# Attention, dense layer and routed experts in one launch: filler matmuls around the routing, and a new order of transposes and low parts in the expert tiles

## The reference

```python
do_compute = (x @ w_skip) > 0            # the other rows pass through
e_idx = np.argmax(xc @ w_gate, axis=1)   # xc: the rows that compute
h = np.maximum(xc[mask] @ w1[e], 0.0)    # 512 -> 1024
y[mask] = gate_w[mask, None] * (h @ w2[e])   # 1024 -> 512
out[do_compute] = xc + y
```

## Time and profile before

| | |
|---|---|
| median of 3 runs | 961.71 us |
| profiled execution | 961.93 us |
| its span | 960.1 us, so 1.8 us lie around it |
| mean granted TensorE clock | 0.959 |
| busy: TensorE, VectorE, ScalarE, GpSimd | 92%, 89%, 69%, 72% |

### The profile page before, as it was taken

The page is one execution under the profiler, slowest core; times in us unless marked ns, Lnnn a source line. Parts: engine busy times, 40 slices in busy tenths (PEclk is TensorE's granted clock), DMA queues, the critical chain, the costliest instruction groups (busy, mean ns, idle before and its releaser), DMA issues.

```text
span 960.1 us, 19356 instructions
## 1 busy us (share of the span) xinstructions
PE 882.6 (92%) x6322; PEld 721.0 (75%) x6322; DVE 854.0 (89%) x1708; ACT 661.8 (69%) x1297; POOL 694.4 (72%) x891
## 2 busy tenths in 40 slices
PE   3566799999999999999999999999999994999996
PEld 1344577888888888888888888888878983777875
DVE  6999999999999998999999999999980237888888
ACT  3677677777787677676778677777764223877875
POOL 2899798877777776787778787778785544566664
PEclk9867699999999999999999999999999995999999
DMA  8964333464354657867436544353343935555970
GB/s 317 376 215 129 118 118 120 157 203 157 115 176 167 192 162 231 241 191 240 136 119 187 169 162 162 127 187 125 132 133 126 333 117 216 200 213 184 337 279 10
DMA packets 69083, 174.76 MB, mean 182 GB/s; under 512 B 20898, under 2 KB 26018, under 8 KB 64624
## 3 DMA queue, kind: packets, MB, share of 16 engines
q1 hardware_dynamic: 67136, 168.39, 52.2%
q0 software_dynamic: 1840, 5.06, 1.6%
HBM read 153.66 MB, written 20.75 MB: 182 GB/s over the span
## 4 chain that ended last, share of the span: by engine, by line
PE 80%; DVE 12%; POOL 2%; issue 2%; ACT 2%; ACTq 0%; DMA 0%; SPq 0%; DVEq 0%; POOLq 0%
PE psum L1188 7%; PE psum L1190 7%; PE psum L1189 7%; PE psum L1128 7%; PE psum L1148 7%; PE psum L1205 7%; PE psum L1206 7%; PE psum L1207 6%; PE psum L1167 6%; DVE top L925 5%; DVE left L931 5%; PE psum L1334 2%; PE psum L1309 2%; PE psum L1131 2%; PE psum L1315 2%
## 5 line engine op out<-in xcount | busy, mean ns | idle before, releaser
L925 DVE MAX8 top<-left 128x8 f32<-128x576 f32 x432 | 305.3, 750 | 0.0
L931 DVE MATCH_REPLACE8 left<-top,left 128x576 f32<-128x576 f32 x288 | 212.1, 745 | 0.0
L565 POOL TENSOR_TENSOR s_sb<-s_sb,below 128x576 f32<-128x576 f32 x144 | 203.3, 1430 | 2.3 <-ACT below L721 2.3
L1188 PE MATMUL psum<-x_high,w_in_high 128*128 128x256 f32 x576 | 169.4, 294 | 1.6 <-POOL x_low L571 1.1
L1190 PE MATMUL psum<-x_high,w_in_low 128*128 128x256 f32 x576 | 163.8, 284 | 0.0
L1189 PE MATMUL psum<-x_low,w_in_high 128*128 128x256 f32 x576 | 163.7, 284 | 0.0
L712 ACT ACTIVATE s_sb<-psum 128x576 f32<-128x576 f32 x144 | 93.5, 650 | 88.6 <-PE psum L1128 72.5
L580 POOL TENSOR_TENSOR square<-relu 128x256 f32<-128x256 f32 x144 | 88.5, 615 | 88.2 <-ACT relu L754 87.7
L1128 PE MATMUL psum<-k_sb,q_sb 64*128 64x288 f32 x512 | 107.2, 499 | 29.6 <-ACT s_sb L712 24.4
L585 POOL TENSOR_TENSOR g_low<-square,g_high 128x256 fp32r<-128x256 f32 x144 | 107.8, 749 | 35.2 <-POOL square L580 27.0
L721 ACT ACTIVATE below<-s_sb,steep_kth 128x576 f32<-128x576 f32 x144 | 110.8, 770 | 29.8 <-POOL neg_max L553 29.8
(11 more groups left out here) (174 smaller groups left out, 1795.3 us busy)
## 6 DMA issues: line engine op xcount, KB each, us to landing
w_ring<-w_split SPq DMA_DIRECT2D x144, 512.0 KB, 4.5
weights<-w SPq DMA_DIRECT2D x32, 1024.0 KB
v_sb<-v_main SPq DMA_DIRECT2D x48, 256.0 KB, 2.6
w_split<-w_ring SPq DMA_DIRECT2D x16, 512.0 KB, 3.8
k_sb<-kT SPq DMA_DIRECT2D x32, 144.0 KB, 4.7
k_sb<-kT SPq DMA_DIRECT2D x32, 128.0 KB, 4.5
q_sb<-qT SPq DMA_DIRECT2D x32, 128.0 KB, 4.3
weights<-w_out SPq DMA_DIRECT2D x1, 4096.0 KB, 13.2
```

The costliest lines, as they stand in the source:

```text
L565: nc.gpsimd.tensor_tensor(s_sb[:, s % SBUFS, n, 0:S], s_sb[:, s % SBUFS, n, 0:S], below[:, n, :], ALU.subtract).then_inc(masked, 1)
L925: v.max(top[:, par, n, r, :], src).then_inc(topk_step, 1)
L931: v.match_replace(left[:, n, :], top[:, par, n, r, :], src, LOWEST).then_inc(topk_step, 1)
L1188: t_.matmul(dst, wh, x_high[:, j % 2, k, :], start=k == 0, stop=False)
```

## The change

It has three parts. `keep_busy(n)` issues n products of 128x128 by 128x512 into PSUM bank 4, which nothing reads; it is called at six places around the routing with 3, 2, 6, 16, 12 and 10. In an expert tile, TensorE transposes hidden half 0 first, then the next tile's rows, then hidden half 1; VectorE makes the low part of w2 piece 2 between the low parts of hidden half 0 and half 1. Before tile 0, VectorE makes the rows' low part ahead of w1 piece 2.

```diff
             def routed_tile(s):            # VectorE
-                for ff in range(3):
-                    split_w2_low(s, at, ff)
+                split_w2_low(s, at, 0)
+                split_w2_low(s, at, 1)
                 place[0] = expert_at(dve, s + 1)
                 for half in range(2):
                     cols = slice(half * 512, (half + 1) * 512)
+                    if half == 1:
+                        split_w2_low(s, at, 2)
                     dve.wait_ge(hT_high_done, 2 * s + half + 1)
...
-            for n in range(3):
-                split_w1_low(0, place[0], n)
+            split_w1_low(0, place[0], 0)
+            split_w1_low(0, place[0], 1)
             split_x_low(0)
+            split_w1_low(0, place[0], 2)
...
+            def keep_busy(n):              # TensorE
+                for _ in range(n):
+                    t_.matmul(psum[:, 4, :], g_high[:, 0, 0:P], g_low[:, 0:2, :].rearrange("p a b -> p (a b)"),
+                              start=True, stop=True)
...
                     if ENDS[j] == t:
+                        if j == GROUPS - 1:
+                            keep_busy(3)
                         transpose_y(j)
                     if ENDS[j] + 1 == t:
+                        if j == GROUPS - 1:
+                            keep_busy(2)
                         route(j)
...
+            keep_busy(6)
             pe.wait_ge(early_sum_set, 1)
             pe.wait_ge(onehot_set, 2)
...
+            keep_busy(16)
             for c in range(NCOL):
                 pe.wait_ge(places_set, 2 if c < EARLY else 3)
...
             last.then_inc(table_done, 1)
+            keep_busy(12)
             pe.wait_ge(meta_set, 2)
...
-                transpose_rows(s + 1)
                 for half in range(2):
+                    if half == 1:
+                        transpose_rows(s + 1)
                     pe.wait_ge(h_done, 2 * s + half + 1)
...
+            keep_busy(10)
             transpose_rows(0)
             each_tile(pe, tiles, MOST, routed_tile)
```

## The result

| | before | after |
|---|---|---|
| median | 961.72 us (6 runs, 961.09 to 963.69) | 966.67 us (6 runs, 966.22 to 967.60) |
| profiled execution, its span | 961.93, 960.1 | 966.28, 964.5 |
| end of the last y in the profile | 955.35 | 960.01 |

The changed kernel is slower by 4.95 us, ratio 1.0047 (95% interval 1.0034 to 1.0060). The forecast was 966.5.

What follows compares the result with a forecast made beforehand. TensorE bounds from tile 1 on at 12.85 us a tile, VectorE and GpSimd close beside. Tile 0 and first tiles -4.5, nine tiles +1.05 each: +4.85 on the profiled 961.93, 0.22 above median, gives 966.5 us (range 957 to 970).

Steps and rivals of the forecast that it cites:

- The case that it falls again: Rival: the clock falls again before tile 0, adding up to 2.1 us, 968.6 us; chance 0.13, with the lock.
- Tile 0: Tile 0's second layer starts at 813.5 and not 817.59, -4.1 us; bounds -2.4 and -4.2.
- 16 products at 0.45: Fillers in the routing at half clock: cost put at 7.3 us, some 3 us more than their wait.
- The transposes: New transpose order on TensorE: -0.38 us per tile, 12.47 a tile, as long as nothing else binds.
- Piece 2 behind L666: VectorE's moved w2 piece 2 meets GpSimd's L666; L660 then precedes w1 piece 1, TensorE gets it 0.9 us late, repeating.
- The round: Time from one tile's end of w1 piece 1 to the next: 13.9 us, +1.05 against 12.85, nine times.
- E: End of VectorE's w1 piece 1 in a tile; TensorE's second layer was to start at E + 5.0.
- its two cases: Who gets the port at w1 piece 0: GpSimd's L660 first, piece 1 done at 13.97; VectorE just ahead, round 13.8.
- the first blow: Tile 1: L666 ends 827.6, L660 holds the port to 833.3, w1 piece 1 ends at 834.4.
- The low parts never reach TensorE: Rival: w1 piece 1 gets the port ahead of L660, -8.3 us, 953.4 us; chance 0.17.
- Only every other tile is hit: Rival: an early L666 lets piece 2 through; five tiles at -0.38, five at +0.6, 958.7 us; chance 0.14.
- The margin at w1 piece 1: In tile time, w1 piece 1's turn at 11.7 against L660's asking at 11.1: 0.6 us.

Runs made afterwards that it cites:

- experiment 11: Kernel with VectorE's tile order put back and L660 waiting for the fourth L868, with six instead of ten fillers in the last call: 952.65 us.
- experiment 9: Kernel with VectorE's tile order put back and L660 waiting for the fourth L868, without the twelve fillers behind the slot table: 954.93 us.
- experiment 2: Kernel before the change with VectorE's new order in the tile alone: 973.13 us against 962.02, ratio 1.0113.
- experiment 4: Kernel before the change with the new order of transposes on TensorE alone: 957.08 us, ratio 0.9951.
- experiment 6: Changed kernel with GpSimd's L660 waiting for the fourth L868 and not the third, so it asks 0.95 us later: 967.22 us, ratio 1.0048.
- experiment 5: Changed kernel with GpSimd's L666 cut to 64 of 512 columns per row from tile 1 on: 951.46 us, ratio 0.9885.
- experiments 3 and 7: Kernel before the change, with the six filler calls alone: 960.65 us; with the rows' low part ahead of w1 piece 2 before tile 0 alone: 960.12 us.

## Why the prediction was right

**The clock and the filler.** As forecast, the clock stays at 1.00 in the changed kernel and in the six other traces that have every call (the last one cut to six in experiment 11). The case that it falls again did not come with pauses of 1.72 to 1.98 us in these seven traces; it came with 4.64 (experiment 9).
The Trainium skill (TensorE: Matmul & The Clock Gate, "What's actually happening") lists the low clock for an idle array. With these pauses the traces agree. In the kernel before the clock fell at 792.5 us, inside a wait of only 1.68 us behind 16 products of 9 columns; idle time alone, as that list has it, does not tell this wait from the 1.98 us through which the clock held.

**Tile 0.** Forecast -4.1 us, measured 4.05 in the profiles. The parts: filler alone 1.4, order alone 2.0, and the new transposes 0.42 (12.85 - 12.43). In the prediction's working 16 products at 0.45 come to 7.2 us and not 7.3; nothing hangs on it.

**The transposes.** Forecast 12.47 a tile and no wait; measured 12.43 to 12.46 where nothing else binds, 4.94 us in all (interval 3.3 to 6.1; forecast for this edit alone 4.4).

**Piece 2 behind L666.** The decisive step held in its parts: w1 piece 1 of tile 1 was to end at 834.4 and ends at 828.80 + 4.56 = 833.36, which is 834.8 with the main part 1.4 us later. The round was forecast at 13.9 and is 14.09. The term mis-sized is the way from E to the second layer, 5.0 in the forecast and 852.60 - 847.45 = 5.15 in the trace: from the start of L1332 to that of the next group are 1.03 us (847.50 to 848.53), and 0.91 in tile 0 (807.16 to 808.07), where no wait stands ahead of it. Of its two cases, 13.97 with GpSimd first and 13.8 with VectorE first, the sum took a value between; the trace has GpSimd first (856.91, VectorE's piece 0 at 857.00). So the tail grew by more than the sum said: from the main part's last product to the end of the last y it was 168.6 us and is 174.7, +6.1, where +4.85 was forecast. By the outputs, tile 0 gave -4.1, tile 1, the first blow, +2.5 (15.3 against 12.85), tiles 2 to 8 +8.8, and tiles 9 and 10, where the kernel before has L660 ahead of w1 piece 1 too, -1.1 (13.66 and 13.62 against 14.77 and 13.65); the forecast had nine equal rounds. The medians moved 4.95 (interval 3.3 to 5.8). That the median came within 0.2 us of 966.5 is partly luck: the tail moved 1.2 us more than forecast, and the medians 1.1 less than the tail. Why is not settled. Single traces stray by this much elsewhere too: tail and medians are +11.9 and +11.1 in experiment 2, -3.4 and -4.9 in experiment 4. The main part's spread of 3 us between executions and a gather that lands up to 1.3 us later are the sizes that would do it, but no run separates them.

**The rivals.** "The low parts never reach TensorE", 953.4 us, is what the kernel does with VectorE's order put back (953.5). "Only every other tile is hit" did not occur: tiles 2 to 8 are all 14.09 to 14.13. The margin at w1 piece 1 was 1.1 us in tile 1 and not 0.6: with tile 1 starting at 817.76, L660 asked 11.1 after it, as forecast, but w1 piece 0 began at 828.80, 11.0 after it (forecast 10.6), because L666 had come at 6.4 (824.17; forecast 5.9). Piece 1's turn was at about 12.2. In experiment 6 L666 came later still (827.43, 6.8 after the tile's start), piece 1's turn with it (12.6), so a request at 12.04 was in time. How thin such margins are shows in experiment 5 (0.26 us on the good side) and in tile 0 of experiment 2 (0.1 us on the bad one).

## What to carry to other kernels

A small operation moved into an engine's idle gap is not free if the operation shares a resource with another engine: read the other engine's row at the new place, and who has asked by the time it is released. Where two engines exclude each other, the delay of one operation (piece 2 takes 2.69 us and not 1.21) can make everything behind it late enough to meet the next exclusion, and a chain of such meetings, not the sum of the work, then sets the period. And of a bundle of edits, time each alone: here -1.4, -2.0, -4.9 and +11.1 us stood behind a +5. They sum to +2.8, not to 5, because the last costs 13.2 us where the others have made the tile shorter: time the bad one in the bundle too.

## What the runs showed of the hardware

Between VectorE's and GpSimd's low parts the one that has asked goes next, and VectorE's waiting operation ends 1.08 to 1.09 us after GpSimd's end in most cases (1.15 at most), not the 1.21 it takes alone. In a few places the order of asking did not decide. VectorE's L1079 of tile 9 starts before GpSimd's L666 in the kernel before, while GpSimd's scatter L692 is still running:

```profile
928.43 5.20 DVE L1079 TENSOR_TENSOR w_low<-weights,w_high 128x1024 fp32r<-128x1024 f32 x2 [0.35 <-ACT w_high L874]
```

```profile
927.85 1.12 POOL L692 DMA_INDIRECT out<-yo,scatter_tab  x1 [0.90 <-DVE yo L1104]
928.98 2.43 POOL L666 TENSOR_TENSOR w_low<-weights,w_high 128x1024 fp32r<-128x1024 f32 x1
```

L666 runs through in 2.43 us, its shortest in this trace, and the first of the two L1079 is held until it is done (931.41). The Trainium skill (SBUF — State Buffer, "SBUF: two separate sides") says that whichever operation starts first gets the port pair for its whole length. Of 432 overlaps of such low parts in the thirteen traces, five do not agree with it, going by the recorded starts: this one, the same tile in experiments 3 and 7 (L1079 from 927.73 and 928.37), and tile 0 in experiments 7 and 9 (from 809.80 and 811.52). In each VectorE's operation starts 0.5 to 0.7 us before GpSimd's, while an indirect DMA of GpSimd's own runs, and takes 4.07 to 4.17 us. Elsewhere VectorE's operations that start during such a DMA go through in 1.2 us, so the DMA alone is not the reason, and which condition is stays open. In tile 0 of the changed kernel's trace the two starts are 0.02 us apart, which is no order.
